# First expert layer of a routed two-layer kernel: one block of 416 slots per expert with the weights stationary, in place of tiles of 128 tokens with the tokens stationary

## The reference, cut to what matters

```
x = attention(q, k, v)                       # 2 x 768 tokens, 8 heads of 64, window 128 and 4 sink tokens -> x (1536, 512)
# layer 1: 8 experts, the best two per token
noisy = x @ w_gate + log1p(exp(x @ w_noise)) * noise
top2, w = the two largest of noisy, softmax over the two
for e in range(8):
    for k in range(2):
        mask = top2[:, k] == e
        out[mask] += w[mask, k] * (relu(x[mask] @ w1[e]) @ w2[e])      # w1 (512, 1024), w2 (1024, 512)
# layer 2: the same shape with its own weights, the best one per token, a bias by modality in the scores
```

## Time and profile before

| | us |
|---|---|
| median of 3 runs (lowest, highest) | 753.37 (753.35, 753.98) |
| profiled execution, first to last instruction (span) | 750.6 |
| what lies around the span (median less span) | 2.8 |
| TensorE busy in the span | 692.2 (92%) |
| layer 1, first expert product to last | 353.2 |
| layer 1's last product to the load of its sum | 7.1 |

### The profile page before, as it was taken

The page is one execution under the profiler, slowest core; times in us unless marked ns, Lnnn a source line. Parts: engine busy times, 40 slices in busy tenths (PEclk is TensorE's granted clock), DMA queues, the critical chain, the costliest instruction groups (busy, mean ns, idle before and its releaser), DMA issues.

```text
span 750.6 us, 14309 instructions
## 1 busy us (share of the span) xinstructions
PE 692.2 (92%) x3683; PEld 566.4 (75%) x3684; DVE 315.6 (42%) x610; ACT 288.0 (38%) x540; POOL 145.3 (19%) x210
## 2 busy tenths in 40 slices
PE   7999999189999999999999999997869999999993
PEld 6889898158888888888888888874637888788872
DVE  3565446665353524425435244221486512442211
ACT  5667667234343414325234143220335412341210
POOL 2400000031222222231312222201042211121101
PEclk9999999589999999999999999999869999999997
DMA  7788430625373634634516322214276711001100
GB/s 207 241 277 285 140 98 29 237 58 197 84 231 77 218 89 127 181 56 140 157 39 211 96 32 53 42 14 113 85 266 250 256 41 56 28 18 43 42 14 24
DMA packets 48865, 91.07 MB, mean 121 GB/s; under 512 B 5055, under 2 KB 11199, under 8 KB 48832
## 3 DMA queue, kind: packets, MB, share of 16 engines
q1 hardware_dynamic: 40320, 69.16, 27.4%
q0 software_dynamic: 8512, 21.50, 12.7%
HBM read 73.61 MB, written 17.56 MB: 121 GB/s over the span
## 4 chain that ended last, share of the span: by engine, by line
PE 85%; DVE 5%; DMA 3%; issue 2%; ACT 2%; SPq 1%; DVEq 0%; ACTq 0%; POOL 0%; POOLq 0%
PE banks L660 11%; PE banks L661 10%; PE banks L665 10%; PE banks L690 10%; PE banks L686 10%; PE banks L687 10%; PE banks L675 5%; PE banks L492 5%; PE banks L520 4%; PE banks L641 2%; PE banks L504 2%; PE banks L551 2%; DMA k_sb<-k_w 1%; DVE row_hot L1144 1%; PE banks L746 1%
## 5 line engine op out<-in xcount | busy, mean ns | idle before, releaser
L879 ACT ACTIVATE hTs<-banks 128x512 fp32r<-128x512 f32 x84 | 50.0, 597 | 313.1 <-PE banks L675 311.0
L660 PE MATMUL banks<-split,xTs 128*128 x336 | 136.5, 406 | 3.1 <-DVE split L988 2.3
L686 PE MATMUL banks<-split,hTs 128*128 x336 | 136.7, 407 | 1.3 <-ACT hTs L879 1.3
L661 PE MATMUL banks<-split,xTs 128*128 x336 | 132.8, 395 | 0.0
L687 PE MATMUL banks<-split,hTs 128*128 x336 | 132.8, 395 | 0.0
L1248 DVE TENSOR_TENSOR hTs<-banks,hTs 128x512 fp32r<-128x512 f32 x84 | 57.8, 690 | 163.8 <-ACT hTs L879 160.0
L988 DVE TENSOR_TENSOR split<-raw,split 128x2048 f32 (+1 forms) x44 | 99.3, 2289 | 52.7 <-ACT split L779 52.4
L690 PE MATMUL banks<-split,hTs 128*128 x336 | 92.4, 396 | 0.4 <-DVE hTs L1248 0.4
L779 ACT ACTIVATE split<-raw 128x2048 f32 (+1 forms) x44 | 82.3, 1907 | 25.9 <-issue 19.6
L665 PE MATMUL banks<-split,xTs 128*128 x336 | 91.8, 394 | 0.0
L443 POOL DMA_INDIRECT x_moe<-rows,dst x28 | 44.6, 1594 | 186.4 <-DVE rows L1256 184.6
(11 more groups left out here) (171 smaller groups left out, 743.9 us busy)
## 6 DMA issues: line engine op xcount, KB each, us to landing
raw<-w1a SPq DMA_DIRECT2D x16, 1024.0 KB
raw<-w2a SPq DMA_DIRECT2D x16, 1024.0 KB
k_sb<-k_w SPq DMA_DIRECT2D x12, 520.0 KB, 4.6
raw<-w1b SPq DMA_DIRECT2D x6, 1024.0 KB
raw<-w2b SPq DMA_DIRECT2D x6, 1024.0 KB
q_sb<-q_t SPq DMA_DIRECT2D x24, 128.0 KB, 3.5
x_attention<-rows SPq DMA_DIRECT2D x12, 256.0 KB, 4.7
split<-x_moe SPq DMA_DIRECT2D x12, 256.0 KB, 5.3
```

The lines of the kernel that those rows point to most:

```text
L660: pe.matmul(psH[:, half, :], xTs[:, 0, c, :], weights(slot, 0, o), start=(c == 0), stop=False)
L661: pe.matmul(psH[:, half, :], xTs[:, 0, c, :], weights(slot, 1, o), start=False, stop=False)
L686: pe.matmul(psY, hTs[:, 0, c, :], weights(slot, 0, o), start=(c == 0), stop=False)
L879: act.activation(hTs[:, 0, half * 4:half * 4 + 4, :].rearrange("p c n -> p (c n)"), psHT[:, half, :], ACT.Copy).then_inc(s["h_high"], 1)
```

## The change

Layer 1 alone is rewritten; attention and layer 2 compute what they did. Each expert has one block of 416 slots (`SLOTS`), 8 blocks in all. The roles of the operands are swapped: a 128x128 piece of the weights is stationary and the 416 slots of the block move. The hidden layer then comes out with features on partitions, so `th` and its 224 transposes in layer 1 go. ACT's relu writes the high part straight out of PSUM, and DVE gets the low part in one operation (`h1_low_part`). The second product comes out turned as well; ACT copies it to `yT`, and `back` (4 transposes for each of 4 pieces) turns it to rows in the midst of the next block's first products. Per block there are 8 x 12 and 4 x 24 products of 416 columns, 16 transposes in (`x1_transposes`) and 16 back.

A block's rows are gathered in four pieces (`SUBS`), the fourth with 32 rows of its own, so the first product of the layer waits for four gathers and four splits, and the 4 products with ones between them are dropped. Gates go through a small DRAM table (`gate_table`), gathered in four pieces per expert. Weight chunks land in the place of their own low part (`stage`), which gives two places, and chunks are asked for a block earlier; expert 1's are asked for after the first gathers instead of during the end of attention. The table of slots has 50 columns instead of 31. Scatters wait only for those two before them. Tokens past an expert's 416th go to tiles of a loop after the eight blocks (`over_layer`), which runs as many times as there are such tiles. The whole layer is written out, not looped.

```diff
+SUBS = 4
+SHORT = 32
+SLOTS = 3 * P + SHORT
+OVER_STEPS = 9
+OVER_TILES = 18
+TABLE = [E * SUBS + OVER_TILES, MOE2_TILES]
...
-            with sp.Fori(1, E) as e:
+            sp.wait_ge(lg_copied, 2 * BLOCKS)
+            for k in range(SUBS):
+                sp.wait_ge(gathered1[k], 16)
+            load_first(sp, 1, 0)
+            load_first(sp, 1, 1)
+            sp.wait_ge(gates_ready, 1)
+            sp.dma_start(gate_table.rearrange("(t p) e -> p t e", p=P), gates8[:]).then_inc(table_stored, 16)
+            load_first(sp, 1, 2)
+            load_first(sp, 1, 3)
+            for e in range(2, E):
+                sp.wait_ge(h1, FC * (e - 1))
                 for c in range(CHUNKS):
+                    if c == 2:
+                        sp.wait_ge(y1, DC * (e - 1))
                     sp.wait_ge(low_done[c], e)
-                    load_chunk(sp, 0, e, c)
+                    load_first(sp, e, c)
...
+            def sub_column(e, k):
+                return SUBS * e + (k + 1) % SUBS
+
+            def gather1(e, k):
+                if e > 0:
+                    pool.wait_ge(tx1, SUBS * (e - 1) + k + 1)
+                col = sub_column(e, k)
+                pool.indirect_dma_start(out=x_rows[:, k], out_offset=None, in_=x_dram[0],
+                                        in_offset=bass.IndirectOffsetOnAxis(ap=src_idx[0][:, col:col + 1], axis=0)
+                                        ).then_inc(gathered1[k], 16)
...
+            def scatter1(e, k):
+                n, col = SUBS * e + k, sub_column(e, k)
+                if k == 0 and e > 0:
                     for b in range(2):
...
+                        pool.wait_ge(scattered1[b], 16 * 2 * e)
+                pool.wait_ge(scaled1, n + 1)
+                pool.indirect_dma_start(out=x_dram[1], out_offset=bass.IndirectOffsetOnAxis(ap=dst_idx[0][:, col:col + 1], axis=0),
+                                        in_=y_room(n), in_offset=None, compute_op=ALU.add, bounds_check=TOK - 1,
+                                        oob_is_err=False).then_inc(scattered1[n % 2], 16)
...
+            def x1_transposes(e, k):
+                pe.wait_ge(gathered1[k], 16 * (e + 1))
...
+            def hidden(psum, slot, f, cols):
+
+                o = (f // 4) * CHUNK + (f % 4) * P
+                for c in range(DC):
+                    pe.matmul(psum, piece(slot, 0, o + c * FH), xTs[:, 0, c, 0:cols], start=(c == 0), stop=False)
+                    pe.matmul(psum, piece(slot, 1, o + c * FH), xTs[:, 0, c, 0:cols], start=False, stop=False)
+                for c in range(DC):
+                    mm = pe.matmul(psum, piece(slot, 0, o + c * FH), xTs[:, 1, c, 0:cols], start=False, stop=(c == DC - 1))
+                return mm
...
+            def first1(e, f):
...
+                    pe.wait_ge(x1_low, SUBS * (e + 1))
+                if n >= 4:
+                    pe.wait_ge(h1_low, n - 3)
+                hidden(psH1[:, f % 4, 0:SLOTS], e % 2, f, SLOTS).then_inc(h1, 1)
+
+            def second1(e, d, between=None):
+                n, psum = DC * e + d, psY1[:, d % 2, 0:SLOTS]
+                if n >= 2:
+                    pe.wait_ge(y1_copied, n - 1)
+                for c in range(FC):
+                    if d == 0:
+                        if c % 4 == 0:
+                            pe.wait_ge(low_done[2 + c // 4], e + 1)
+                        pe.wait_ge(h1_high, FC * e + c + 1)
+                    o = DC * F + c * D + d * P
+                    pe.matmul(psum, piece(e % 2, 0, o), hTs[:, 0, c, :], start=(c == 0), stop=False)
+                    pe.matmul(psum, piece(e % 2, 1, o), hTs[:, 0, c, :], start=False, stop=False)
+                if between is not None:
+                    x1_transposes(e + 1, between)
+                for c in range(FC):
+                    if d == 0:
+                        pe.wait_ge(h1_low, FC * e + c + 1)
+                    mm = pe.matmul(psum, piece(e % 2, 0, DC * F + c * D + d * P), hTs[:, 1, c, :], start=False, stop=(c == FC - 1))
+                mm.then_inc(y1, 1)
+
+            def back(e, k, psum):
...
+                first = min(k * P, SLOTS - P)
+                for d in range(DC):
+                    mm = pe.transpose(psum[:, d * P:(d + 1) * P], yT[:, d, first:first + P], ident[:])
+                mm.then_inc(rows1, 1)
...
+            route(0)
+            pe.wait_ge(slots_ready[0], 1)
+            for k in range(SUBS):
+                x1_transposes(0, k)
+            for e in range(E):
+                for f in range(FC):
+                    first1(e, f)
+                    if e > 0 and f % 2 == 0:
+                        if e > 1 or f > 0:
+                            pe.wait_ge(scaled1, SUBS * (e - 1) + f // 2)
+                        back(e - 1, f // 2, psO1)
+                for d in range(DC):
+                    more = e < E - 1
+                    second1(e, d, {1: 1, 2: 3}.get(d) if more else None)
+                    if more and d < 2:
+                        x1_transposes(e + 1, 2 * d)
+            for k in range(SUBS):
+                pe.wait_ge(scaled1, SUBS * (E - 1) + k - (k > 0))
+                back(E - 1, k, (psO1, psX1)[k % 2])
+            pe.sem_inc(over_y, 1)
...
+            def relu1(e, f):
+                act.wait_ge(h1, FC * e + f + 1)
+                act.activation(hTs[:, 0, f, :], psH1[:, f % 4, 0:SLOTS], ACT.Relu).then_inc(h1_high, 1)
...
+            def y1_copy(e, d):
+                act.wait_ge(y1, DC * e + d + 1)
+                if e > 0 and d == 0:
+                    act.wait_ge(rows1, SUBS * e)
+                act.activation(yT[:, d, :], psY1[:, d % 2, 0:SLOTS], ACT.Copy).then_inc(y1_copied, 1)
...
+                    link(dve.scalar_tensor_tensor(start[:], start[:], float(P), over_base[:], ALU.mult, ALU.add))
+                    dve.wait_ge(pe_route, 2)
+                    link(dve.scalar_tensor_tensor(ra[:], ranks, float(SLOTS), spread(start[:], 1, TILES), ALU.is_ge, ALU.mult))
+                    link(dve.tensor_tensor(place[:], ranks, spread(expert_base[:], 1, TILES), ALU.add))
+                    link(dve.tensor_tensor(place[:], place[:], ra[:], ALU.add))
...
+            def h1_low_part(e, f):
+                dve.wait_ge(h1_high, FC * e + f + 1)
+                dve.scalar_tensor_tensor(hTs[:, 1, f, :], psH1[:, f % 4, 0:SLOTS], 0.0, hTs[:, 0, f, :].bitcast(F32),
+                                         ALU.max, ALU.subtract).then_inc(h1_low, 1)
+
+            def y_scale(e, k):
...
+                dve.tensor_scalar(x_rows[:, k] if last else y_rows[:, n % 2], (psO1, psX1)[k % 2] if last else psO1,
+                                  sub_gate[:, e % 2, k, e:e + 1], None, ALU.mult).then_inc(scaled1, 1)
+
...
+                for e in range(E):
+                    more = e < E - 1
+                    for f in range(FC):
+                        h1_low_part(e, f)
+                        if e > 0 and f % 2 == 0:
+                            y_scale(e - 1, f // 2)
+                        if more and f in (1, 4):
+                            first_layer_low(e + 1, f // 4)
+                    if more:
+                        for k in range(SUBS):
+                            x1_low_part(e + 1, k)
+                        for c in (2, 3):
+                            first_layer_low(e + 1, c)
+                for k in range(SUBS):
+                    y_scale(E - 1, k)
...
-                keep_clock_up(REST_FIRST[m])
```

More of the change, by code:

```diff
@@ L102, in build @@
         h_sb = rows[:, 4:6, :].rearrange("p a n -> p (a n)")
[L103 to L114, removed]
+        x_rows = rows[:, 0:SUBS, :]
+        y_rows = rows[:, SUBS:6, :]
+        xT = sb("xT", [P, DC, P])
         ident = sb("ident", [P, P])
@@ new lines, in scatter @@
+            def scatter(t, b, half):
+                if not isinstance(half, int) or half > 0:
+                    gated(pool, "pool", scattered[b], half * 16)
+                if isinstance(t, int) and t == 0:
+                    pool.wait_ge(dst_ready, 2)
+                pool.tensor_copy(dst1[:, b:b + 1], dst_idx[1][:, bass.ds(t, 1)]).then_inc(dst_copied, 1)
+                gated(pool, "pool", dst_copied, t + 1)
+                gated(pool, "pool", y_copied, t + 1)
+                where = bass.IndirectOffsetOnAxis(ap=dst1[:, b:b + 1], axis=0)
+                pool.indirect_dma_start(out=out, out_offset=where, in_=y_sb[:, b], in_offset=None,
+                                        bounds_check=TOK - 1, oob_is_err=False).then_inc(scattered[b], 16)
@@ new lines, in _ @@
+            for t in range(3):
+                gather(t, t % 2)
+            for b in range(2):
+                gather(b + 3, 1 - b)
+                scatter(b, b, 0)
+            with pool.Fori(1, LEAST2 // 2 - 1) as r:
+                for b in range(2):
+                    gather(r * 2 + (b + 3), 1 - b)
+                    scatter(r * 2 + b, b, r)
+            pool.wait_ge(fresh_ready[1], 1)
```

(26 more changed lines are left out.)

740 lines of the change are left out of this document (466 added, 274 removed).

## The result

The changed kernel takes **728.57 us** (725.76 to 731.67, 4 runs), the kernel before 753.36 beside it; the ratio is 0.9671, 95% interval 0.9638 to 0.9704. That is 24.8 us less. The forecast was 16.3 us less, 737.1, in a range of 729 to 750: the sign was right and the size was not, and the time fell 0.4 us outside the range. The profiled execution spans 726.2 us against 750.6, 24.4 less.

A forecast was written before the change was run, and what follows sets the result against it. TensorE alone was taken to bound layer 1. Layer 1 -30.3, start +7.7 and end +6.3 sum to -16.3 us, from 753.37 to 737.1 us, with a range of 729 to 750 for 8 in 10.

The forecast's parts named there:

- a transpose costs 0.110: Layer 1 on TensorE: 0.110 us per transpose, 224 between first and last product, 24.6 us instead of 37.0.
- all splits, copies and scatters stay hidden: DVE, ACT and GpSimd work in layer 1 counted at nothing: 20, 17 and 16 us per block of 40 us.
- the start: Ahead of layer 1: first product 7.7 us later, mostly three more gathered pieces waiting on one bank, 6.45 us.
- the end: Last product of layer 1 to the load of the sum: 13.5 us instead of 7.1, taken as 6.3 longer.
- weight-load rival: Layer 1: the weight load sets the 0.2333 us pace, so fewer columns save nothing; 801.5 us, slower, chance 0.10.
- overflow: After the blocks: a token past 416 adds a whole expert load and 192 products, some 40 us each; chance 0.01.
- the pace: Layer 1 products of 416 columns: 0.1914 us start to start instead of 0.2333 at 512; 1536 make 294.0 us.
- my two ends: Pace at 416 columns in layer 1: 0.1896 us if the extra scales with columns, 0.1933 if it is fixed.
- the third piece's transposes: Layer 1, each block: PE's third piece of transposes waits about 0.1 us for its bank, 1 us in all.
- the clock: First products of layer 1: TensorE's clock expected at half, 1.2 GHz, costing 3.3 us.
- my -30.3: Layer 1 as a whole: 322.9 us against 353.24, from products, transposes, bank waits and clock.
- layer 2 at nothing: Layer 2 keeps its instructions and shifts as a whole, with no change in time.

The follow-up runs named there:

- 256-column run: Changed kernel with 256 columns instead of 416 in 1440 of layer 1's 1536 products, its results left incomplete; 649.68 us.
- widths of 256 and 448: Changed kernel with 256 columns in nearly all layer 1 products, 649.68 us; changed kernel with blocks of 448 slots instead of 416, 750.6 us.
- padding runs: 32 bytes put ahead of the stationary operands in the kernel before, 745.16 us; ahead of layer 2's alone in the changed kernel, 731.36 us.
- kernel before with padding: Kernel before with 32 bytes ahead of its turned tokens and hidden rows, and 32 behind, so they begin at multiples of 64 bytes; 745.16 us.

## Why the prediction was right in its sign and short in its size

**Right.** TensorE alone is the bound of layer 1 before and after; the products go from 512 columns to 416 and get faster; a transpose costs 0.110; all splits, copies and scatters stay hidden; the start waits on one bank, 7.7 forecast and 8.6 measured (0.45 us more per piece, at the lower clock, where I had put 0.3 in all; the routing ahead of it gave 0.6 back); the end 6.3 forecast (its own 13.5 less 7.1 makes 6.4), 6.5 measured. The weight-load rival, my only way to a slower kernel besides an overflow, is refuted by the 256-column run.

**The step that failed: the pace.** I read 0.2333 as one number, columns plus an extra of 20 ns, asked only whether that extra scales, and took the middle of 0.1896 and 0.1933. It was two things. About 4 ns of it are the price of operands that begin at 32 past a multiple of 64 bytes, which the change happened to remove. The rest is an extra of 15.7 ns at 512 columns that measured 15.3 at 416. From the aligned 0.229 my two ends would have been 0.1861 and 0.1890; the measured 0.1886 lies between them, near the fixed one, and below both of the ends that I had. That the extra is fixed is not shown by this; the widths of 256 and 448 speak against it. 1,536 products at 2.8 ns below my value make 4.3 us. Two smaller terms go the same way: 1.0 us for the third piece's transposes did not show, and the clock cost 1.9, not 3.3. Together 6.7, of which the layer shows 5.5. The 1.2 left over is time that none of my terms has: with the measured values they add up to 316.2 of the layer's 317.42. The kernel before has 2.6 of it too (313.6 + 37.0 = 350.6 of 353.24), which my -30.3 let vanish without a reason.

The Trainium skill, "TensorE: Matmul & The Clock Gate", Part 2 (back-to-back issue gap), gives columns / 2.4 GHz plus 2.5 ns for the isolated gap and names no type; that it holds for every type, as the prediction has it, was my reading. By it 416 columns would be 175.8 ns; the trace has 188.6 for fp32r, and the aligned 512 columns 229 instead of 215.8. Its Part 3 (what overlaps) lets a load overlap only when the row group differs; the 256-column run contradicts this, with a full load per product every 0.118 us.

**The second step that failed: layer 2 at nothing.** The instructions were the same, as I said; the addresses were not. Layer 2 gave 2.8 us, and the padding runs move 2.3 and 2.5 us there and back. Of the change's 24.8 us, 7.5 to 8.1 are the address, by the median and by the ratio of the kernel before with padding. What is left for the change itself is (0.9892 - 0.9671) x 753.4 = 16.6 us, give or take 3.5 by the two intervals. That is close to the 16.3 forecast, in part because the other misses cancel.

**Not foreseen and not explained.** From layer 2's last product to the end 12.6 us became 10.0. It repeats: 12.6 in both profiles of the kernel before and with its padding, 10.0 in the changed one and all its variants. The rows of the line that closes the program show where it lies, before and after (duration in ns, then the start in us):
```profile
L55 POOLq DRAIN  x1: 6932/6932/6932, 743.5 to 743.5; - x1
...
L62 POOLq DRAIN  x1: 4032/4032/4032, 722.0 to 722.0; - x1
```
GpSimd's last instruction, a drain behind its last scatter, takes 6.93 us before and 4.03 after, 2.9 less; what stands ahead of it takes 0.3 more. Why it is shorter stays open: no run was aimed at it. Scoring and the second routing are 1.7 us longer; for scoring the granted clock, 0.79 against 0.83 in the earlier trace rows, goes with 1.0 of it. Together these two take 0.9 us off that no term of the prediction had.

## What to carry to other kernels

Before costing a product's pace, compare the same instruction elsewhere in the trace and look at where its operands begin: a change of tensor sizes can move everything that is allocated after it, and with it the pace of code that nobody touched. Where moving tokens replace moving weights, the gain is columns at 2.4 GHz plus transposes saved; an extra per product stays, and so does the price of padding, here 21.9 / 32 = 0.7 us for each slot that all eight experts get more. Batching four gathers ahead of the first product needs as many landing banks as the gathers' pace asks for (here two), and something to keep TensorE busy between them.

## What the runs showed of the hardware

- fp32r products of 416 to 512 columns start 15.3 to 16.3 ns later than their columns at 2.4 GHz, products of 256 columns 11 ns; bf16 of 512 columns 3 ns.
- An operand of such products at 32 past a multiple of 64 bytes costs 3.5 to 4.4 ns per product of 512 columns, whether it is the loaded or the moving one (2.6 us over layer 2 when the weights moved, 2.5 when the tokens were loaded), and 1.8 to 3.7 us over a layer of 1,536 products of 416 columns. Bf16, other offsets and other engines were not tried.
- Full float32 weight loads fit under products 0.118 us apart, though each has a record of 188 ns.
- Gathers issued 1.27 us apart fed transposes 1.2 to 1.8 us apart; issuing four scatters back to back took 1.85 us each.
- GpSimd's drain at the end of the kernel took 6.93 us in the kernel before and 4.03 in the changed one, the same in every profile of either; the runs do not say why.
